# x times w_in2 by seven products of 2x2 blocks, and w_out2's parts from DRAM through a ring

## The chip, the cores and the metric
One Trainium2 chip, one of its cores. The metric is the device time of the kernel in microseconds. The engines are TensorE (PE; its weight loads are shown as PEld), VectorE (DVE), ScalarE (ACT), GpSimd (POOL) and SyncE (SP), which here issues all DMAs.

## The reference
```
attention, twice, for 8 batches x 8 heads (seq 576, head_dim 64, 32 packs):
    p_packed = softmax(p k^T / 8) v ;  a = softmax(q p_packed^T / 8) p_packed
x  = a, heads side by side                      (4608 tokens x 512)
h  = x @ w_in1 ;  g = h - tanh(h) ;             x1 = g @ w_out1   (512 -> 2048 -> 512)
h2 = x1 @ w_in2 ; g2 = s*relu(h2)^2 + b ;       y  = g2 @ w_out2  (512 -> 2048 -> 512)
```
All in float32. x1 and y are kept transposed, features on the partitions.

## The kernel before, in words
Every large product is made of three matmuls (`product`, lines 172 to 176). Each operand is split into a high part (rounded to the type in which TensorE takes a column per cycle) and a low part (the rest), and high*high, high*low and low*high are added up in PSUM. Each of the three brings its own 128 x 128 weights.

The work has two layers. The first (batches 0 to 7, two units of 288 tokens each, 16 units) holds the attention and the first pair of weights. The attention's second half is folded into the weights: m parts (`MB`) are the packed values times w_in1. A unit has 16 steps, one per chunk of 128 hidden features: `first1` makes the chunk (6 matmuls of 288 columns), ScalarE and VectorE make g and its two parts, and two steps later `second` multiplies them with w_out1 into four banks (12 matmuls). `side` puts the attention's small matmuls for the next batch behind fixed steps; step m counts 0 to 31 in a batch, and the loops of ScalarE and VectorE have the same steps written out. x1 goes to DRAM unit by unit (`store_x`).

The second layer has 9 blocks of 512 tokens, 16 steps each, 144 steps. A block's x1 is read back (`load_x`), and GpSimd splits it into parts (`split_x`), two blocks in turn. `first2` makes a chunk of h2 from the four row blocks of w_in2: 4 x 3 matmuls of 512 columns. ScalarE does relu (L656), VectorE the square (L923), ScalarE scale and bias (L659) and the high part (L663), VectorE the low part (L927). `second` multiplies with w_out2, 12 matmuls of 512 columns, two steps behind. All of w_in2 and w_out2 lies in SBUF as parts: w_in2 is loaded in batch 7 and split by ScalarE and VectorE, one piece of 512 columns per step (`high_w_in2`, `low_w_in2`); w_out2 is loaded into w_out1's place as that comes free, and GpSimd splits it (`split_w_out`).

The order on each engine is the program's order, and semaphores join them. TensorE's loop is

```
for c in range(STEPS + LAG):
    if c < STEPS1:
        first1(c)
        side(c)
    elif c < STEPS:
        first2(c)
    if c >= LAG:
        second(c - LAG)
```

Banks 0 to 3 hold the output of `second`, banks 4 and 5 the chunks of h in turn, banks 6 and 7 the attention's work.

## Time and profile before

| | us |
|---|---|
| median of 3 runs | 1506.68 (1506.4 to 1507.57) |
| the profiled execution | 1507.28, its span 1505.5 |
| TensorE busy | 1492.1 |
| VectorE busy | 642.9 |
| ScalarE busy | 611.7 |
| GpSimd busy | 158.0 |
| DMA, mean over the span | 50 GB/s, 75.43 MB |

The busy time of an engine adds up the time in which at least one of its instructions runs. Matmuls overlap, so the mean duration of one is longer than the time it adds. The first layer ends and the second begins at about 715 us of the span.

### The profile page before, as it was taken

Reading aid. Unit: us, or ns where it says so; the run is one execution under the profiler, and the core shown is the slowest. Engines: PE = TensorE matmul, PEld = TensorE weight load, DVE = VectorE, ACT = ScalarE, POOL = GpSimd, SP = SyncE. Lnnn points to the kernel's source line nnn. Section 1 sums busy time; section 2 is a strip of 40 time slices with the busy share of each in tenths; the row PEclk is TensorE's granted clock in tenths of the full one; section 3 lists DMA queues with packets and bytes.
Section 4 is the critical chain, followed back from the end, with each engine's and each line's share of the span. In section 5 each row is a group of like instructions: output and inputs, shape, how many; then the busy total and the mean of one; then the engine's idle time right before and its main releaser. Section 6 shows DMA issues by size and latency. Waiting matters only on the chain.

```text
span 1505.5 us, 23375 instructions
## 1 busy us (share of the span) xinstructions
PE 1492.1 (99%) x9852; PEld 1300.5 (86%) x9852; DVE 642.9 (43%) x1212; ACT 611.7 (41%) x1185; POOL 158.0 (10%) x95
## 2 busy tenths in 40 slices
PE   7999999999999999999999999999999999999999
PEld 5999989898998989899888888888888888888887
DVE  5755555555555555565333223232322323232222
ACT  3444344444444444454434333343334334333333
POOL 4600000000000000003912002020200202020000
PEclk9999999999999999999999999999999999999999
DMA  9402121120212110033201001010101001010000
GB/s 347 144 17 80 48 80 49 48 67 15 80 49 79 49 48 17 2 129 126 75 1 56 0 6 51 1 57 0 56 1 24 32 1 56 1 57 0 28 1 28
DMA packets 48888, 75.43 MB, mean 50 GB/s; under 512 B 1936, under 2 KB 26640, under 8 KB 48784
## 3 DMA queue, kind: packets, MB, share of 16 engines
q1 hardware_dynamic: 48784, 73.93, 14.9%
q8 instruction: 79, 1.29, 0.4%
q14 instruction: 25, 0.20, 0.0%
HBM read 55.05 MB, written 18.87 MB: 49 GB/s over the span
## 4 chain that ended last, share of the span: by engine, by line
PE 99%; DVE 1%; DMA 0%; issue 0%; ACT 0%; SPq 0%; DVEq 0%
PE banks L174 32%; PE banks L175 31%; PE banks L176 31%; PE banks L402 2%; PE banks L351 1%; PE banks L373 1%; PE banks L417 1%; PE banks L359 0%; DMA kT<-k_T 0%; PE banks L341 0%; PE banks L382 0%; PE banks L360 0%; DVE m_parts L733 0%; DVE g_low L888 0%; DVE probs L750 0%
## 5 line engine op out<-in xcount | busy, mean ns | idle before, releaser
L174 PE MATMUL banks<-g_high,w_out_parts 128*128 128x288 f32 (+1 forms) x1600 | 534.0, 334 | 1.3 <-DVE m_parts L733 1.3
L176 PE MATMUL banks<-g_high,w_out_parts 128*128 128x288 f32 (+1 forms) x1600 | 525.7, 329 | 0.0
L175 PE MATMUL banks<-g_low,w_out_parts 128*128 128x288 f32 (+1 forms) x1600 | 525.5, 328 | 0.0
L174 PEld LDWEIGHTS banks<-g_high,w_out_parts 128*128 128x128 f32 x1600 | 300.0, 187 | 62.3 <-issue 37.9
L175 PEld LDWEIGHTS banks<-g_low,w_out_parts 128*128 128x128 f32 x1600 | 300.4, 188 | 22.6
L176 PEld LDWEIGHTS banks<-g_high,w_out_parts 128*128 128x128 f32 x1600 | 300.3, 188 | 22.4
L923 DVE TENSOR_TENSOR g<-banks,g 128x512 f32<-128x512 f32 x144 | 99.6, 692 | 331.6 <-ACT g L656 331.6
L656 ACT ACTIVATE g<-banks 128x512 f32<-128x512 f32 x144 | 86.1, 598 | 366.3 <-PE banks L176 366.3
L176 PE MATMUL banks<-x_parts,w_in_parts 128*128 128x512 f32 x576 | 224.1, 389 | 0.0
L174 PE MATMUL banks<-x_parts,w_in_parts 128*128 128x512 f32 x576 | 224.1, 389 | 0.0
L175 PE MATMUL banks<-x_parts,w_in_parts 128*128 128x512 f32 x576 | 224.1, 389 | 0.0
L608 ACT ACTIVATE g<-banks 128x288 f32<-128x288 f32 x256 | 105.2, 411 | 287.0 <-PE banks L176 285.9
L847 DVE TENSOR_TENSOR g<-banks,g 128x288 f32<-128x288 f32 x256 | 117.1, 457 | 227.2 <-ACT g L608 226.0
L927 DVE TENSOR_TENSOR g_low<-g,g_high 128x512 fp32r<-128x512 f32 x144 | 118.8, 825 | 221.1 <-ACT g_high L663 221.1
L659 ACT ACTIVATE g<-g,small 128x512 f32<-128x512 f32 x144 | 117.5, 816 | 109.3 <-DVE g L923 109.3
L174 PE MATMUL banks<-probs2T_parts,m_parts 128*128 128x288 f32 x512 | 151.9, 297 | 5.4 <-DVE probs2T_parts L774 5.4
L292 POOL TENSOR_TENSOR x_parts<-x_raw,small 128x2048 fp32r<-128x2048 f32 (+1 forms) x12 | 33.0, 2747 | 1167.5 <-DMA x_raw<-x1T_scratch 1167.5
L629 ACT CAST g_high<-g 128x288 fp32r<-128x288 f32 x256 | 110.7, 433 | 101.5 <-DVE g L847 100.3
L888 DVE TENSOR_TENSOR g_low<-g,g_high 128x288 fp32r<-128x288 f32 x256 | 125.1, 489 | 62.4 <-ACT g_high L629 60.0
L175 PE MATMUL banks<-probs2T_parts,m_parts 128*128 128x288 f32 x512 | 151.7, 296 | 0.0
L176 PE MATMUL banks<-probs2T_parts,m_parts 128*128 128x288 f32 x512 | 151.0, 295 | 0.0
L176 PEld LDWEIGHTS banks<-x_parts,w_in_parts 128*128 128x128 f32 x576 | 108.1, 188 | 22.6
(85 smaller groups left out, 1188.9 us busy)
## 6 DMA issues: line engine op xcount, KB each, us to landing
kT<-k_T SPq DMA_DIRECT2D x16, 576.0 KB, 4.5
qT<-q_T SPq DMA_DIRECT2D x16, 576.0 KB, 6.0
x1T_scratch<-x_store SPq DMA_DIRECT2D x16, 576.0 KB, 3.4
x_raw<-x1T_scratch SPq DMA_DIRECT2D x9, 1024.0 KB, 6.5
v_rows<-v_rows SPq DMA_DIRECT2D x8, 1024.0 KB, 5.3
w_out_raw<-w_out SPq DMA_DIRECT2D x8, 1024.0 KB, 9.3
out_T<-y_store SPq DMA_DIRECT2D x8, 1024.0 KB, 8.7
w_in_rows<-w_in SPq DMA_DIRECT2D x4, 1024.0 KB, 13.2
```

Source lines behind the costliest of these rows:

```text
L174: nc.tensor.matmul(out, high, rhigh, start=first, stop=False)
L175: nc.tensor.matmul(out, high, rlow, start=False, stop=False)
L176: return nc.tensor.matmul(out, low, rhigh, start=False, stop=last)
L292: return nc.gpsimd.tensor_tensor(high, raw, ones, ALU.mult)
L608: nc.scalar.activation(TG1[:, c % 2, :], HB[:, c % 2, 0:U1], ACT.Tanh).then_inc(act_done, 1)
L629: nc.scalar.copy(GH1[:, c % RING, :], TG1[:, c % 2, :]).then_inc(high_done, 1)
L656: nc.scalar.activation(TG2[:, c % 2, :], HB[:, c % 2, :], ACT.Relu).then_inc(act_done, 1)
L659: nc.scalar.activation(TG2[:, c % 2, :], TG2[:, c % 2, :], ACT.Identity, bias=b_col, scale=s_col).then_inc(g_done, 1)
L847: nc.vector.tensor_tensor(TG1[:, c % 2, :], HB[:, c % 2, 0:U1], TG1[:, c % 2, :], ALU.subtract).then_inc(g_done, 1)
L888: nc.vector.tensor_tensor(GL1[:, c % RING, :], TG1[:, c % 2, :], read(GH1[:, c % RING, :]), ALU.subtract).then_inc(low_done, 1)
L923: nc.vector.tensor_tensor(TG2[:, c % 2, :], HB[:, c % 2, :], TG2[:, c % 2, :], ALU.mult).then_inc(r2_done, 1)
L927: nc.vector.tensor_tensor(GL2[:, c % RING, :], TG2[:, c % 2, :], read(GH2[:, c % RING, :]), ALU.subtract).then_inc(low_done, 1)
```

## The change
In the second layer, h2 = x1 w_in2 is computed by Strassen's scheme in Winograd's form on 2 x 2 blocks: w_in2 is cut into two halves of the contraction (256 rows each) by pairs of chunks (128 hidden features each), a block of x1 into the same two halves by two halves of its tokens (256 each). `seven` makes the seven products of a pair of chunks, each 2 x 3 matmuls of 256 columns, where two steps had 2 x 12 of 512. Products 1 to 4 go to the left halves of banks 4 to 7, 5 to 7 to the right halves of banks 4 to 6; each waits until its bank has been read. ScalarE copies product 1; VectorE adds the others up to the four blocks of h2 (c11, c12, c21, c22) and makes relu(h)*h in one operation per chunk.

The sums and differences of the blocks are made ahead and split: of w_in2 once, for each of 8 pairs of chunks (`mix_w_in2`, `high_w_in2`, `low_w_in2`), from step 5 of batch 7 to the fourth pair of the second layer; of x1 for each of the 9 blocks, by VectorE and ScalarE (`mix_x` at the fifth pair of the block before, `high_x` and `low_x` at its last), no longer by GpSimd. TensorE's order is seven(0), then seven(Q) ahead of the two `second2` of pair Q-1.

The parts of w_in2's combinations take w_out2's room. w_out2 is split by GpSimd through a staging tile, three chunks per batch in batches 1 to 6, and its parts are stored to DRAM. In the second layer a ring of four chunks (512 KB each) is refilled by SyncE, one chunk per step, each time a chunk has been used.

```diff
+PF = FC // 2
+U2H = U2 // 2
+NPR = 7
+PAIRS2 = NU2 * PF
...
+MIX_AT = {5: 0, 12: 1, 15: 2, 18: 3, 26: 4, 30: 5}
+SPLIT_AT = {7: (0, 0), 10: (0, 1), 13: (1, 0), 14: (1, 1), 16: (2, 0), 17: (2, 1), 19: (3, 0), 20: (3, 1),
+    27: (4, 0), 28: (4, 1), 31: (5, 0)}
+X_AT = {23: (0, 1), 25: (2, 3), 29: (4,), 30: (5,)}
+MIX2_AT = {0: 6, 2: 7}
+SPLIT2_AT = {0: ((5, 1),), 1: ((6, 0), (6, 1)), 2: ((7, 0),), 3: ((7, 1),)}
...
+    w2_dram = nc.dram_tensor("w_out2_parts_scratch", (FC, P, 2 * DM), F32).ap()
...
+    def split_w_out2(i):
+        wait(sp, w_out2_out, 16 * i)
+        sp.dma_start(STG_RAW[:, 1, :], w_out2[i, :, :]).then_inc(w_out2_raw_in, 16)
+        sp.wait_ge(w_out2_split, i + 1)
+        sp.dma_start(w2_dram[i, :, :].rearrange("p (a f) -> p a f", a=2), read(STG[:, :, :])
+                     ).then_inc(w_out2_out, 16)
+
+    def second_done(c):
+        unit, i = divmod(c, FC)
+        if i < FC - 1:
+            sp.wait_ge(g_used, (FC - 1) * unit + i + 1)
+        else:
+            sp.wait_ge(o_done, KX * (unit + 1))
+
+    def load_w_out2(cc):
+        sp.dma_start(read(WR[:, cc % RING, :, :]), w2_dram[cc % FC, :, :].rearrange("p (a f) -> p a f", a=2)
+                     ).then_inc(w_out2_in[cc % RING], 16)
+
...
+            for q in range(PF // 2):
+                load_w_in2(q)
+            sp.wait_ge(s2_done, NU1)
+            sp.wait_ge(x1_out, 32)
+            load_x(0)
...
+        if 1 <= b < B - 1:
+            for i in range(3 * b - 3, min(3 * b, FC)):
+                split_w_out2(i)
...
+    sp.wait_ge(w_out2_out, 16 * FC)
+    second_done(STEPS1 - FC + 1)
+    for cc in range(RING):
+        load_w_out2(cc)
+    for q, i in ((4, 5), (5, 8), (6, 12), (7, 15)):
+        second_done(STEPS1 - FC + i)
+        load_w_in2(q)
...
+    for Q in range(PAIRS2):
+        n, q = divmod(Q, PF)
+        if q == 0 and n + 1 < NU2:
+            sp.wait_ge(xo_ready, NPR * (n + 1))
+            load_x(n + 1)
+        for cc in (2 * Q + RING, 2 * Q + RING + 1):
+            if cc < 2 * PAIRS2:
+                second_done(STEPS1 + cc - RING)
+                load_w_out2(cc)
+        if q == 1 and n >= 1:
+            sp.wait_ge(o_copied_act, 2 * (NU1 + n))
+            sp.wait_ge(o_copied_dve, 2 * (NU1 + n))
+            sp.dma_start(outT[:, (n - 1) * U2:n * U2].rearrange("(d p) t -> p d t", p=P),
...
-        split_x(n)
+        pool.wait_ge(w_out2_raw_in, 16 * (i + 1))
+        split(STG[:, 0, :], STG[:, 1, :], STG_RAW[:, 1, :], 2 + FC + i + 1, w_out2_split)
...
+    def seven(Q):
+
+        n, q = divmod(Q, PF)
+        for j in range(NPR):
+            if n == 0:
+                pe.wait_ge(wc_ready, 2 * q + 1 + j // 4)
+            if q == 0:
+                pe.wait_ge(xo_ready, NPR * n + j + 1)
+            if j == 4:
+                pe.wait_ge(p1_copied, Q + 1)
+            elif j > 4:
+                pe.wait_ge(comb_done, NPR * Q + j - 4)
+            elif Q >= 1:
+                pe.wait_ge(comb_done, NPR * (Q - 1) + (4, 5, 7, 6)[j])
+            elif j == 0:
+                pe.wait_ge(g_done, STEPS1)
+            elif j == 2:
+                pe.wait_ge(dve_max2, 2 * (NU1 - 1))
+            out = banks[:, 4 + j % 4, (j // 4) * U2H:(j // 4 + 1) * U2H]
+            w = WC[q // 4][:, q % 4, j, :, :]
+            for kp in range(2):
+                cols = slice(kp * P, (kp + 1) * P)
+                last = product(out, w[:, 0, cols], w[:, 1, cols], XO[:, j, 0, kp, :], XO[:, j, 1, kp, :],
+                               kp == 0, kp == 1)
+            last.then_inc(prod_done, 1)
+
+    def second2(cc):
+
+        n, i = divmod(cc, FC)
+        pe.wait_ge(low_done, STEPS1 + cc + 1)
+        pe.wait_ge(w_out2_in[cc % RING], 16 * (cc // RING + 1))
+        for d in range(KX):
+            if i == 0:
+                pe.wait_ge((o_copied_act, o_copied_dve)[d % 2], 2 * (NU1 + n) - 1 + d // 2)
+            cols = slice(d * P, (d + 1) * P)
+            last = product(O[:, d, :], WR[:, cc % RING, 0, cols], WR[:, cc % RING, 1, cols],
+                           GH2[:, cc % RING, :], GL2[:, cc % RING, :], i == 0, i == FC - 1)
...
+    seven(0)
+    for Q in range(1, PAIRS2 + 1):
+        if Q < PAIRS2:
+            seven(Q)
+        second2(2 * Q - 2)
+        second2(2 * Q - 1)
...
+    def high_w_in2(q, part):
+        act.wait_ge(wc_mix, 4 * q + 3 + part)
+        rows = slice(0, 4) if part == 0 else slice(4, NPR)
+        nc.scalar.copy(WC[q // 4][:, q % 4, rows, 0, :], WC_RAW[q // 4][:, q % 4, rows, 1, :]
+                       ).then_inc(wc_high, 1)
+
+    def high_x(n, j):
+        if j in (0, 1, 4):
+            act.wait_ge(x_in, 16 * (n + 1))
+        else:
+            act.wait_ge(xt_done, 4 * n + {3: 1, 5: 2, 2: 3, 6: 4}[j])
+        if n == 0:
+            act.wait_ge(h_done, STEPS1 - FC + 4 * (j // 2) + 4)
+        else:
+            act.wait_ge(prod_done, NPR * (PF * n - 1) + j + 1)
+        nc.scalar.copy(XO[:, j, 0, :, :], x_raw(j)).then_inc(xo_high, 1)
...
+    high_x(0, 6)
     act.wait_ge(sb_in, 32)
...
+    for Q in range(PAIRS2):
...
+        act.wait_ge(prod_done, NPR * Q + 1)
+        if Q >= 1:
+            act.wait_ge(comb_done, NPR * (Q - 1) + 2)
+        nc.scalar.copy(C1[:, :], banks[:, 4, 0:U2H]).then_inc(p1_copied, 1)
+
+        if q == PF - 1 and n + 1 < NU2:
+            for j in range(NPR):
+                high_x(n + 1, j)
+
+        for k in range(2):
+            cc = 2 * Q + k
+            act.wait_ge(r2_done, cc + 1)
+            nc.scalar.activation(TG2[:, k, :], TG2[:, k, :], ACT.Identity, bias=b_col, scale=s_col
+                                 ).then_inc(g_done, 1)
+            act.wait_ge(g_done, STEPS1 + cc + 1)
+            nc.scalar.copy(GH2[:, cc % RING, :], TG2[:, k, :]).then_inc(high_done, 1)
+
+        for f, part in SPLIT2_AT.get(Q, ()):
+            high_w_in2(f, part)
...
+    def mix_w_in2(q):
+        w = WC_RAW[q // 4][:, q % 4, :, 1, :]
+        dve.wait_ge(wc_in[q], 32)
+        nc.vector.tensor_tensor(w[:, 3, :], w[:, 5, :], w[:, 6, :], ALU.add).then_inc(wc_mix, 1)
+        nc.vector.tensor_tensor(w[:, 5, :], w[:, 0, :], w[:, 5, :], ALU.subtract).then_inc(wc_mix, 1)
+        dve.wait_ge(wc_mix, 4 * q + 1)
+        nc.vector.tensor_tensor(w[:, 2, :], w[:, 3, :], w[:, 0, :], ALU.subtract).then_inc(wc_mix, 1)
+        dve.wait_ge(wc_mix, 4 * q + 3)
+        nc.vector.tensor_tensor(w[:, 4, :], w[:, 1, :], w[:, 2, :], ALU.subtract).then_inc(wc_mix, 1)
+
+    def low_w_in2(q, part):
+        dve.wait_ge(wc_high, 2 * q + part + 1)
+        dve.wait_ge(wc_mix, 4 * q + 4)
+        rows = slice(0, 4) if part == 0 else slice(4, NPR)
+        nc.vector.tensor_tensor(WC[q // 4][:, q % 4, rows, 1, :], WC_RAW[q // 4][:, q % 4, rows, 1, :],
+                                read(WC[q // 4][:, q % 4, rows, 0, :]), ALU.subtract).then_inc(wc_ready, 1)
...
+            wait(dve, xo_high, NPR * n)
+            nc.vector.tensor_tensor(TR[:, 0, :, :], b12, b11, ALU.subtract).then_inc(xt_done, 1)
+            nc.vector.tensor_tensor(TR[:, 1, :, :], b22, b12, ALU.subtract).then_inc(xt_done, 1)
+        else:
+            dve.wait_ge(xt_done, 4 * n + 1)
+            nc.vector.tensor_tensor(TR[:, 2, :, :], b22, TR[:, 0, :, :], ALU.subtract).then_inc(xt_done, 1)
+            dve.wait_ge(xt_done, 4 * n + 3)
+            nc.vector.tensor_tensor(TR[:, 3, :, :], TR[:, 2, :, :], b21, ALU.subtract).then_inc(xt_done, 1)
...
+    def low_x(n, j):
+        dve.wait_ge(xo_high, NPR * n + j + 1)
+        nc.vector.tensor_tensor(XO[:, j, 1, :, :], x_raw(j), read(XO[:, j, 0, :, :]), ALU.subtract
+                                ).then_inc(xo_ready, 1)
...
+        elif m in (21, 22):
+            mix_x(0, m - 21)
+        elif m in MIX_AT:
+            mix_w_in2(MIX_AT[m])
...
+        else:
+            if m in SPLIT_AT:
+                low_w_in2(*SPLIT_AT[m])
+            for j in X_AT.get(m, ()):
+                low_x(0, j)
...
+    low_x(0, 6)
+    for Q in range(PAIRS2):
...
+        dve.wait_ge(prod_done, own + 2)
+        dve.wait_ge(p1_copied, Q + 1)
+        plus(c11, C1[:, :], half(5, 0))
+        dve.wait_ge(prod_done, own + 3)
+        plus(u2, C1[:, :], half(6, 0))
+        dve.wait_ge(prod_done, own + 4)
+        dve.wait_ge(comb_done, own + 2)
+        plus(c12, u2, half(7, 0))
+        dve.wait_ge(prod_done, own + 5)
+        dve.wait_ge(comb_done, own + 3)
+        plus(c12, c12, half(4, 1))
+        dve.wait_ge(comb_done, own + 4)
+        if Q >= 1:
+            dve.wait_ge(high_done, STEPS1 + 2 * Q - 1)
+        nc.vector.scalar_tensor_tensor(TG2[:, 0, :], C[:, 0, :], 0.0, C[:, 0, :], ALU.max, ALU.mult
+                                       ).then_inc(r2_done, 1)
+        dve.wait_ge(prod_done, own + 6)
+        plus(u3, u2, half(5, 1))
+        dve.wait_ge(comb_done, own + 5)
+        plus(c22, u3, half(7, 0))
+        dve.wait_ge(prod_done, own + 7)
+        plus(c21, u3, half(6, 1), ALU.subtract)
+        dve.wait_ge(comb_done, own + 7)
+        if Q >= 1:
+            dve.wait_ge(high_done, STEPS1 + 2 * Q)
+        nc.vector.scalar_tensor_tensor(TG2[:, 1, :], C[:, 1, :], 0.0, C[:, 1, :], ALU.max, ALU.mult
+                                       ).then_inc(r2_done, 1)
+
+        if Q in MIX2_AT:
+            mix_w_in2(MIX2_AT[Q])
+        last_pair = q == PF - 1 and n + 1 < NU2
+        if last_pair:
+            low_x(n + 1, 0)
+            low_x(n + 1, 1)
+        low_g(2 * Q)
+        if last_pair:
+            low_x(n + 1, 2)
+            low_x(n + 1, 3)
+        low_g(2 * Q + 1)
+        if last_pair:
+            for j in (4, 5, 6):
+                low_x(n + 1, j)
+        for f, part in SPLIT2_AT.get(Q, ()):
+            low_w_in2(f, part)
+        if q == PF // 2 and n + 1 < NU2:
+            mix_x(n + 1, 0)
+            mix_x(n + 1, 1)
```

## Rows read from the trace of the kernel before

**Rows 1.** Page: busy time of engines; chain that ended last, by engine
```profile
PE 1492.1 (99%) x9852; PEld 1300.5 (86%) x9852; DVE 642.9 (43%) x1212; ACT 611.7 (41%) x1185; POOL 158.0 (10%) x95
...
PE 99%; DVE 1%; DMA 0%; issue 0%; ACT 0%; SPq 0%; DVEq 0%
```

**Rows 2.** Waits of TensorE: who waited for whom, us in total, times, longest
```profile
PE banks L174 <- DVE probs2T_parts L774: 5.4, 1, 5.4
PE banks L174 <- DVE m_parts L733: 1.3, 1, 1.3
```

**Rows 3.** Timeline (start us, duration us), ScalarE: first, last of 25, of 128
```profile
654.34 0.41 ACT L608 ACTIVATE g<-banks 128x288 f32<-128x288 f32 x1 [1.03 <-PE banks L176]
...
711.70 0.41 ACT L608 ACTIVATE g<-banks 128x288 f32<-128x288 f32 x1 [1.03 <-PE banks L176]
...
803.28 0.60 ACT L656 ACTIVATE g<-banks 128x512 f32<-128x512 f32 x1 [2.62 <-PE banks L176]
...
1494.16 0.60 ACT L656 ACTIVATE g<-banks 128x512 f32<-128x512 f32 x1 [2.62 <-PE banks L176]
```

**Rows 4.** Timeline of TensorE: after a break, and transposes
```profile
306.16 0.19 PEld L174 LDWEIGHTS banks<-g_high,w_out_parts 128*128 128x128 f32 x1 [0.47 <-issue]
306.16 0.40 PE L174 MATMUL banks<-g_high,w_out_parts 128*128 128x288 f32 x1
306.27 0.19 PEld L175 LDWEIGHTS banks<-g_low,w_out_parts 128*128 128x128 f32 x1
...
141.05 0.60 PE L359 MATMUL banks<-identity,probs 128*128 128x128 f32 x4
141.48 0.27 PE L360 MATMUL banks<-identity,probs 128*64 128x128 f32 x1
```

**Rows 5.** VectorE by line, shape: busy us, mean ns, idle before, releaser
```profile
L927 DVE TENSOR_TENSOR g_low<-g,g_high 128x512 fp32r<-128x512 f32 x144 | 118.8, 825 | 221.1 <-ACT g_high L663 221.1
...
L923 DVE TENSOR_TENSOR g<-banks,g 128x512 f32<-128x512 f32 x144 | 99.6, 692 | 331.6 <-ACT g L656 331.6
...
L824 DVE TENSOR_TENSOR w_in_parts<-w_in_raw,w_in_parts 128x512 fp32r<-128x512 f32 x16 | 10.8, 677 | 0.0
...
L741 DVE TENSOR_TENSOR m_parts<-banks,m_parts 128x256 fp32r<-128x256 f32 x1 | 0.4, 418 | 0.0
```

**Rows 6.** ScalarE by line and shape
```profile
L659 ACT ACTIVATE g<-g,small 128x512 f32<-128x512 f32 x144 | 117.5, 816 | 109.3 <-DVE g L923 109.3
...
L663 ACT CAST g_high<-g 128x512 fp32r<-128x512 f32 x144 | 89.3, 620 | 4.5
...
L551 ACT COPY probs<-banks 128x288 f32<-128x288 f32 x14 | 5.5, 392 | 0.0
```

**Rows 7.** Timeline of VectorE in batch 7: two operations in a row
```profile
676.65 0.68 DVE L824 TENSOR_TENSOR w_in_parts<-w_in_raw,w_in_parts 128x512 fp32r<-128x512 f32 x1
677.25 0.45 DVE L888 TENSOR_TENSOR g_low<-g,g_high 128x288 fp32r<-128x288 f32 x1
```

**Rows 8.** Timeline near 1000 us: GpSimd and VectorE
```profile
997.86 4.94 POOL L306 TENSOR_TENSOR x_parts<-x_raw,x_parts 128x2048 fp32r<-128x2048 f32 x1
...
1001.99 1.37 DVE L927 TENSOR_TENSOR g_low<-g,g_high 128x512 fp32r<-128x512 f32 x1 [1.54 <-ACT g_high L663]
```

**Rows 9.** Window: PE, PEld, DVE, ACT, POOL busy us (count); clock, DMA, GB/s
```profile
25.00:60.00 35.00, 33.56 (x293) 28.79 (x286) 28.59 (x44) 16.30 (x39) 33.58 (x27) 0.97 0.73 255
```

**Rows 10.** DMA issues: size, us to landing; w_in2's four loads, their landing
```profile
x1T_scratch<-x_store SPq DMA_DIRECT2D x16, 576.0 KB, 3.4
x_raw<-x1T_scratch SPq DMA_DIRECT2D x9, 1024.0 KB, 6.5
...
out_T<-y_store SPq DMA_DIRECT2D x4, 256.0 KB, 2.0
...
644.27 3.21 SPq L207 DMA_DIRECT2D w_in_raw<-w_in  x4
...
DMA to landing us min/median/max: 6.5/9.4/12.2
```

More of the change, by code:

```diff
@@ L141, in build @@
     w_in1_in = [sem(f"w_in1_in{i}") for i in range(NB)]
[L142 removed]
+    wc_in = [sem(f"w_in2_in{q}") for q in range(PF)]
     w_out1_in = [sem(f"w_out1_in{i}") for i in range(4)]
[L144 to L145 removed]
+    w_out2_in = [sem(f"w_out2_in{i}") for i in range(RING)]
+    w_out2_raw_in, w_out2_split, w_out2_out = sem("w_out2_raw_in"), sem("w_out2_split"), sem("w_out2_out")
+    x_in = sem("x_in")
     zeroed, ident_ready = sem("zeroed"), sem("ident_ready")
@@ L176, in product, with x_raw @@
         return nc.tensor.matmul(out, low, rhigh, start=False, stop=last)
+    def x_raw(j):
+        if j in (0, 1, 4):
+            kh, th = ((0, 0), (1, 0), None, None, (1, 1))[j]
+            return XR[:, 2 * kh:2 * kh + 2, th * U2H:(th + 1) * U2H]
+        return TR[:, {3: 0, 5: 1, 2: 2, 6: 3}[j], :, :]
     block = nc.Block()
@@ L225, in _ @@
             load_w_in1(0)
-            load_w_out(0, w_out1, w_out1_in)
+            load_w_out1(0)
             load_w_in1(1)
@@ L247, in _ @@
                     sp.wait_ge(m_done, NB * B)
-                    for k in range(KX):
-                        load_w_in2(k)
+                    for q in range(PF // 2):
[3 more added lines that the diff above has]
+                    load_x(0)
                 if b + 2 < B:
@@ L438, in first1, with second1 @@
                 last.then_inc(h_done, 1)
-            def first2(c):
-                n, i = divmod(c - STEPS1, FC)
-                if i == 0:
-                    pe.wait_ge(xb_ready, KX + n)
-                if c == STEPS1:
-                    pe.wait_ge(w_in2_ready, KX * NB)
-                pe.wait_ge(g_done, c - 1)
-                for k in range(KX):
-                    cols = slice(k * FF + i * P, k * FF + (i + 1) * P)
-                    last = product(HB[:, c % 2, :], WIN[:, 0, cols], WIN[:, 1, cols],
-                                   XB[:, n % 2, 0, k, :], XB[:, n % 2, 1, k, :], k == 0, k == KX - 1)
-                last.then_inc(h_done, 1)
-            def second(c):
+            def second1(c):
                 unit, i = divmod(c, FC)
-                width, ring_high, ring_low, ready = (U1, GH1, GL1, w_out1_ready) if c < STEPS1 else \
-                    (U2, GH2, GL2, w_out2_ready)
                 pe.wait_ge(low_done, c + 1)
-                pe.wait_ge(ready, i + 1)
+                pe.wait_ge(w_out1_ready, i + 1)
                 if c == 0:
@@ L466, in second @@
                     cols = slice(d * P, (d + 1) * P)
-                    last = product(O[:, d, 0:width], WOUT[:, 0, i, cols], WOUT[:, 1, i, cols],
-                                   ring_high[:, c % RING, :], ring_low[:, c % RING, :], i == 0, i == FC - 1)
+                    last = product(O[:, d, 0:U1], WOUT[:, i, 0, cols], WOUT[:, i, 1, cols],
+                                   GH1[:, c % RING, :], GL1[:, c % RING, :], i == 0, i == FC - 1)
+                    if i == FC - 1:
+                        last.then_inc(o_done, 1)
+                    elif d == KX - 1:
+                        last.then_inc(g_used, 1)
@@ L528, in _ @@
             m_block(0, 0)
-            for c in range(STEPS + LAG):
+            for c in range(STEPS1 + LAG):
                 if c < STEPS1:
@@ new lines, in half, with plus, low_g @@
+            def half(b, h):
+                return banks[:, b, h * U2H:(h + 1) * U2H]
+            def plus(out, a, p, op=ALU.add):
+                nc.vector.tensor_tensor(out, a, p, op).then_inc(comb_done, 1)
+            def low_g(cc):
+                dve.wait_ge(high_done, STEPS1 + cc + 1)
+                nc.vector.tensor_tensor(GL2[:, cc % RING, :], TG2[:, cc % 2, :], read(GH2[:, cc % RING, :]),
+                                        ALU.subtract).then_inc(low_done, 1)
+            low_x(0, 6)
@@ new lines, in _ @@
+            for Q in range(PAIRS2):
+                n, q = divmod(Q, PF)
+                own = NPR * Q
+                if Q == 0:
+                    for d in (1, 3):
+                        copy_o(NU1 - 1, d, OS1, U1, x1_out, 16 * (NU1 - 1))
+                if q == 1 and n >= 1:
+                    for d in (1, 3):
+                        copy_o(NU1 + n - 1, d, OS2, U2, y_out, 16 * (n - 1))
+                c11, c12, c21, c22 = (C[:, k, h * U2H:(h + 1) * U2H] for k in range(2) for h in range(2))
+                u2, u3 = U[:, 0, :], U[:, 1, :]
+                dve.wait_ge(prod_done, own + 2)
[44 more added lines that the diff above has]
+                    mix_x(n + 1, 1)
```

182 lines of the change are left out of this document (67 added, 115 removed).

## The prediction
> **What bounds the kernel now.** I read the page first: TensorE is busy 99% of the span and 99% of the chain that ended last runs through it [rows 1]. The waits of TensorE add up to 10.9 us, the two longest are 5.4 and 1.3 us, and by the lines that end them all belong to the first layer [rows 2]. So a change counts by what it does to TensorE's own time, unless it makes TensorE wait. What one matmul costs there is not its busy mean (matmuls overlap) but its slot, the distance to the next one. It is read from the rhythm of ScalarE's first operation on each step, which starts when a step's hidden columns are done [rows 3]. In the first layer 24 steps take 57.36 us, 2.390 us each; a step has 6 + 12 matmuls of 288 columns, so a slot is 0.1328 us. In the second layer 127 steps take 690.88 us, 5.440 us each for 12 + 12 matmuls of 512 columns: 0.2267 us. Both are 0.013 us above the time of the columns at the granted 2.4 GHz (0.120 and 0.2133 us).
>
> **TensorE's work after the change.** The unit is a pair of chunks (two steps). Before, a pair is 48 matmuls of 512 columns, 10.88 us; the half that multiplies with w_out2 stays (24, 5.44 us). The other half becomes 7 products x 2 halves of the contraction x 3 parts = 42 matmuls of 256 columns. No row of the second layer shows this width. The line through the two slots of rows 3 has (0.2267 - 0.1328)/224 = 0.00042 us per column and gives 0.1328 - 32 x 0.00042 = 0.1194 us. 42 x 0.1194 = 5.01 us against 5.44: 0.43 us less per pair, and over 72 pairs 30.7 us less.
> That is small, since 18 more slots pay the fixed 0.013 us, and it hangs on the slot. Upper bound: every matmul here brings its own weights, and if 0.1328 were the least that a weight load allows, 42 slots would take 5.58 us, 9.9 us more over the kernel than before. Lower bound: after a break in the first layer two weight loads start 0.11 us apart, with no matmul ahead of them, and four transposes with 128 columns and 128 weights each follow each other every 0.108 us [rows 4]; a slot as short as 0.110 us gives 4.62 us, 59 us less over the kernel. I take the line: 0.1194 lies above what rows 4 need for the weights, and the excess over the columns was the same at both widths.
> The Trainium skill ("TensorE: Matmul & The Clock Gate", section "Back-to-back issue gap") has columns / 2.4 + 2.5 ns for the slot, which would be 0.109 us here and a saving of 61 us instead of 30.7. The trace disagrees at both widths that it has: 0.1328 against the rule's 0.1225 and 0.2267 against 0.2158 [rows 3]. Its figure for a load of 128 weights (same page, "LDWEIGHTS (loading the stationary operand)") is 107 ns, and there the trace agrees with 0.11 us [rows 4].
>
> **The other engines, per pair.** VectorE now forms h from the products: 7 operations on 256 columns at about 0.42 us, two squares with relu on 512 columns (an operation that no row shows; between 0.68 and 0.83 us by the two-input operations of that width, I take 0.69, the row that reads PSUM, as it is also what an undisturbed row of the SBUF form takes), and two low parts at 0.69 [rows 5]. One that waits for nothing starts 0.08 us before the last one's end [rows 7]. That is 5.0 to 5.7 us in a pair of 10.45. ScalarE copies the first product (0.37 us by the copy of 288 columns), and twice scales (0.82) and casts (0.62): 3.3 us [rows 6]. The relu on ScalarE goes. GpSimd's splits of x go with the whole second layer's use of it: a low part beside one took 1.37 us instead of 0.69 [rows 8]. None of this was on TensorE's path, so it counts nothing.
>
> **Waits inside a pair.** Count from the end of a pair's seven products, T. A product is seen about 0.19 us after its last slot (its last matmul outlasts its slot by about 0.16). Product 5 writes the bank of product 1 and waits for ScalarE's copy; product 6 waits for c11, product 7 for u2. Product 2 is seen 1.6 us after the seven begin, c11 is done at 2.05, product 6 is due at 3.6: 1.5 us to spare, if VectorE is free. It is: after T the order is u3, c22, c21 (to T+1.05), the second square (T+1.8), ScalarE's scale and cast of it (T+3.3), low parts (T+2.4 to 4.3). The next seven begin at T+5.44, since the 24 matmuls with w_out2 lie between. At the fifth pair of a block (512 tokens) four mixes of x follow, 2.7 us, to T+7: still ahead of T+8.6, when c11 must start.
> At the last pair of a block seven high parts (ScalarE) and seven low parts (VectorE) of the next x are added. ScalarE follows the products: 0.62 against 0.72 us each, the last one at T+0.8. VectorE's order is u3, c22, c21, square, two low x, low g, two, low g, three; at 0.6 to 0.69 us each it ends at T+7.2, then c11 at T+7.6, due T+9.0. The low parts are due from T+5.4 on, one every 0.72 us, and come from T+2.4 on. I count nothing; without the overlap of rows 7 and with the 0.83 us mean of the low parts [rows 5] it would be T+9.4 for the low parts, and c11 0.8 us late, at 8 edges.
> The start of the layer has no such cover: seven(1) follows seven(0) at once. ScalarE finishes the casts of pair 0 at T+3.25 and one weight split (768 columns, about 0.8 us), only then copies product 1: done T+4.4 where product 5 is due at T+2.9, 1.6 us lost. VectorE has the second square, four mixes of w_in2, two low parts and a weight split (about 0.9): c11 at T+5.8, due 5.2, 0.6 us lost. 2.2 us once.
>
> **Work moved into the first layer.** Batch 7 had 16 high and 16 low parts of w_in2 of 512 columns; now VectorE has 5 mixes of four 256-column operations before step 27 (about 1.5 us each), splits of 1024 and 768 columns (1.2 and 0.9), mixes and low parts of x. Between steps 12 and 23, the densest, this is 15 us beside 9 us of its own work, in 28.7 us of TensorE's. It fits; I allow 0.5 us for a step that is late. The splits of w_out2 go to batches 1 to 6, sixteen times two GpSimd operations. In the stretch where GpSimd did the same for w_out1 (27 operations in 35 us) VectorE's 44 operations took 0.65 us each, longer than alone, yet TensorE was busy 33.56 of 35 us, and the 1.3 us wait in it is for an m part [rows 9, 2]. SyncE stops at each split, 2.0 us of load for 256 KB, two GpSimd operations at 33.58/27 = 1.24 us, 3.4 of store for 512 to 576 KB, 8 us, 24 for three [rows 9, 10]. Only the store of x of that batch is queued behind; it goes out near step 27 instead of 17, and its buffer is written again at step 33, 14 us later. Nothing.
>
> **The ring.** Each chunk's 512 KB goes out when the chunk four before it is used, and it is due 2.72 + 5.01 + 5.44 + 5.01 = 18.2 us later. Beside it the queue holds at worst one more chunk and a transfer of 1 MB. Four loads of 1 MB issued within 3.2 us landed 6.5 to 12.2 us after their issue, one x load took 6.5 [rows 10]. So 2 MB is there in about 9 us, and the ring hides. Its 75 MB make about 100 GB/s over the layer; the start had 255 GB/s beside matmuls [rows 9].
>
> **Sum.** The profiled execution took 1507.28 us, 1.78 more than its span and 0.6 more than the median. 1507.28 - 30.7 + 2.2 + 0.5 = 1479.3; by the median 1478.7. I say 1479.
>
> **Rivals.**
> (a) VectorE is late at the block edges or by one operation more in each pair, because the unseen square or the waits between dependent operations are dearer. 1 to 2 us at 8 edges make 1487 to 1495. For it: the mean of 0.83 us. Against: it contains GpSimd's share, which goes. 19%.
> (b) The slot has a floor of 0.1328 us from its own weights. 9.9 + 2.7 us over before: 1519. For it: no row has a shorter slot of this kind. Against: the 0.11 us of rows 4, and the same excess at 512 columns, where weights can't bind. 6%.
> (c) The chain product 2, c11, product 6 is late in each pair, from behind VectorE's earlier work. It decides from 1.5 us of delay on and eats the gain from 0.43 us of stall per pair, 1.9 us of delay; at 1 us of stall it is 1479 + 72 = 1551. Against: VectorE is about half idle. Slower than before 5%, in part (1496 to 1505) 4%, at no change 2%.
> (d) A slot near 0.110 us, which the weights allow: 1507 - 59 + 2.7 = 1451. Against: the constant excess. 4%.
> The Trainium skill's slot rule (same page and section as above) would put it there too, at 1449; the trace does not follow it.
> (e) The ring is late: from 18 us of landing on each microsecond counts per chunk. It belongs with (c) by size, and rows 10 leave it half of that; it is in (c)'s share.
>
> **The numbers.** Forecast 60% (1475 to 1484), rivals as given. Faster by over 0.2% (3 us, about what a measurement of this kernel can tell): 60 + 19 + 4 + 4 = 87%; within 2%; slower 6 + 5 = 11%. The range takes forecast and (a): 1473 to 1496.
>
> **What would show it.** Right: a pair lasts 10.45 us in steady state, by the starts of ScalarE's copy of product 1; the 256-column matmuls start 0.119 us apart; TensorE's waits name VectorE's c11 or ScalarE's copy at pair 1 alone, some 2 us; GpSimd is still after batch 6; batches 1 to 6 keep their length. Wrong: slots of 0.13 us between the seven; waits on the combining lines every pair or every eighth pair; low x waits; a wait on the ring's loads.

## The result: 1482.18 us, 1.7% less, and the profile after

The changed kernel takes 1482.18 us (median of 4 runs, 1481.46 to 1482.29) where the kernel before took 1507.12 beside it (4 runs, 1506.40 to 1508.70). The ratio is 0.9832, with a 95% interval of 0.9815 to 0.9849. The forecast was 1479. The profiled execution took 1481.46 us with a span of 1479.7, 25.8 us less than before in both.

Busy time of the engines on the page after, against [rows 1]:

```profile
PE 1463.2 (99%) x11148; PEld 1337.7 (90%) x11148; DVE 902.5 (61%) x1847; ACT 594.8 (40%) x1176; POOL 79.9 (5%) x71
```

VectorE has 260 us more to do and the kernel is faster: TensorE is as full as before, and its own time fell by 28.9 us.

The rhythm is read as in [rows 3], now from ScalarE's copy of product 1, of which each pair of chunks has one. These are the copies of pair 3 and pair 71 (counted from 0) in the timeline after:

```profile
747.28 0.37 ACT L752 COPY p_copy<-banks 128x256 f32<-128x256 f32 x1 [2.17 <-PE banks L204]
...
1461.28 0.37 ACT L752 COPY p_copy<-banks 128x256 f32<-128x256 f32 x1 [3.12 <-PE banks L204]
```

714.00 us for 68 pairs are 10.50 us each, against 10.88 for two steps before. Every one of the 68 is 10.50: no block edge, no fifth pair stands out.

The slot of the new width, from TensorE's timeline after (first, tenth after it):

```profile
999.80 0.28 PE L202 MATMUL banks<-x_operands,w_in_first 128*128 128x256 f32 x1
...
1001.00 0.28 PE L203 MATMUL banks<-x_operands,w_in_first 128*128 128x256 f32 x1
```

Ten slots are 1.20 us: 0.120 us each. The waits of TensorE after, with those that answer to [rows 2] first:

```profile
PE banks L202 <- DVE probs2T_parts L871: 5.4, 1, 5.4
PE banks L202 <- DVE m_parts L830: 1.7, 1, 1.7
PE banks L202 <- ACT p_copy L752: 1.4, 1, 1.4
...
PE banks L202 <- DVE h L1060: 0.4, 1, 0.4
```

Two waits are new, each once. The timeline at the start of the second layer shows them in order (SyncE's, VectorE's low parts and TensorE's other rows left out):

```profile
719.01 0.37 ACT L752 COPY p_copy<-banks 128x256 f32<-128x256 f32 x1 [0.72 <-PE banks L204]
...
726.28 0.83 ACT L664 CAST w_in_last<-w_in_raw_last 128x768 fp32r<-128x768 f32 x1
...
727.02 0.36 ACT L752 COPY p_copy<-banks 128x256 f32<-128x256 f32 x1
...
727.47 0.95 DVE L934 TENSOR_TENSOR w_in_last<-w_in_raw_last,w_in_last 128x768 fp32r<-128x768 f32 x1
...
727.53 0.36 PE L202 MATMUL banks<-x_operands,w_in_first 128*128 128x256 f32 x1 [1.36 <-ACT p_copy L752]
...
728.33 0.41 DVE L1060 TENSOR_TENSOR h<-p_copy,banks 128x256 f32<-128x256 f32 x1
...
728.89 0.35 PE L202 MATMUL banks<-x_operands,w_in_first 128*128 128x256 f32 x1 [0.42 <-DVE h L1060]
...
736.78 0.37 ACT L752 COPY p_copy<-banks 128x256 f32<-128x256 f32 x1 [0.89 <-PE banks L204]
```

ScalarE's copy of pair 1 (727.02) starts right behind the weight split (726.28), and TensorE's product 5 behind the copy. The price of both waits is read from the copies of pairs 0 and 2: they are 736.78 - 719.01 = 17.77 us apart. Without a wait the distance would be 42 slots for the seven products of pair 1, which follow those of pair 0 at once, and then one ordinary pair: 5.04 + 10.50 = 15.54. The waits cost 2.2 us.

VectorE's operations after, by line and shape, against [rows 5]:

```profile
L1064 DVE TENSOR_TENSOR g_low<-g,g_high 128x512 fp32r<-128x512 f32 x144 | 98.9, 688 | 58.1 <-ACT g_high L764 58.1
...
L1105 DVE SCALAR_TENSOR_TENSOR g<-h 128x512 f32<-128x512 f32 x72 | 50.0, 694 | 2.4
...
L1060 DVE TENSOR_TENSOR h<-p_copy,banks 128x256 f32<-128x256 f32 x72 | 30.4, 422 | 149.3 <-PE banks L204 149.3
```

The low part fell from a mean of 825 to 688 ns, with GpSimd still. In the trace before, the 22 of its 144 low parts that had an operation of GpSimd beside them took 1561 ns on average, the other 122 took 692: the mean of [rows 5] was high through those 22 alone. The unseen square takes 694.

### The profile page after: what moved, and what is told of

It is laid out like the page before. It is cut to its first block, busy times and chain, and to the rows that moved or that the text cites. A ratio compares the mean times of both kernels' runs of the same rounds, so it can differ in the third digit from the quotient of the medians.

```text
span 1479.7 us, 27233 instructions
## 1 busy us (share of the span) xinstructions
PE 1463.2 (99%) x11148; PEld 1337.7 (90%) x11148; DVE 902.5 (61%) x1847; ACT 594.8 (40%) x1176; POOL 79.9 (5%) x71
## 4 chain that ended last, share of the span: by engine, by line
PE 97%; DVE 2%; DMA 0%; ACT 0%; issue 0%; SPq 0%; DVEq 0%
PE banks L202 31%; PE banks L203 31%; PE banks L204 30%; PE banks L442 2%; PE banks L413 1%; PE banks L391 1%; PE banks L457 1%; PE banks L399 1%; DMA kT<-k_T 0%; DVE g_low L1020 0%; DVE m_parts L830 0%; PE banks L422 0%; PE banks L400 0%; DVE probs L900 0%; DVE h L1060 0%
## 5 line engine op out<-in xcount | busy, mean ns | idle before, releaser
L202 PE MATMUL banks<-g_high,w_out_parts 128*128 128x288 f32 x1024 | 309.9, 303 | 1.7 <-DVE m_parts L830 1.7
L204 PE MATMUL banks<-g_high,w_out_parts 128*128 128x288 f32 x1024 | 301.6, 295 | 0.0
L203 PE MATMUL banks<-g_low,w_out_parts 128*128 128x288 f32 x1024 | 301.4, 294 | 0.0
L202 PEld LDWEIGHTS banks<-g_high,w_out_parts 128*128 128x128 f32 x1024 | 192.0, 187 | 40.2 <-issue 33.6
L202 PE MATMUL banks<-g_high,w_out_ring 128*128 128x512 f32 x576 | 225.0, 391 | 0.0
L203 PE MATMUL banks<-g_low,w_out_ring 128*128 128x512 f32 x576 | 224.9, 391 | 0.0
L204 PE MATMUL banks<-g_high,w_out_ring 128*128 128x512 f32 x576 | 224.1, 389 | 0.0
L204 PEld LDWEIGHTS banks<-g_high,w_out_parts 128*128 128x128 f32 x1024 | 192.3, 188 | 0.0
L203 PEld LDWEIGHTS banks<-g_low,w_out_parts 128*128 128x128 f32 x1024 | 192.2, 188 | 0.0
L1020 DVE TENSOR_TENSOR g_low<-g,g_high 128x288 fp32r<-128x288 f32 x256 | 129.9, 507 | 66.1 <-ACT g_high L718 63.9
L202 PE MATMUL banks<-x_operands,w_in_first 128*128 128x256 f32 x504 | 142.6, 283 | 1.8 <-ACT p_copy L752 1.4
L204 PE MATMUL banks<-x_operands,w_in_last 128*128 128x256 f32 x504 | 142.6, 283 | 0.0
L204 PE MATMUL banks<-x_operands,w_in_first 128*128 128x256 f32 x504 | 142.6, 283 | 0.0
L203 PE MATMUL banks<-x_operands,w_in_last 128*128 128x256 f32 x504 | 142.6, 283 | 0.0
L203 PE MATMUL banks<-x_operands,w_in_first 128*128 128x256 f32 x504 | 142.6, 283 | 0.0
```

The lines of the kernel that those rows point to most:

```text
L202: nc.tensor.matmul(out, high, rhigh, start=first, stop=False)
L203: nc.tensor.matmul(out, high, rlow, start=False, stop=False)
L204: return nc.tensor.matmul(out, low, rhigh, start=False, stop=last)
L1020: nc.vector.tensor_tensor(GL1[:, c % RING, :], TG1[:, c % 2, :], read(GH1[:, c % RING, :]), ALU.subtract).then_inc(low_done, 1)
```

## The experiments

**The ring alone.** The kernel before, with w_out2 split in batches 1 to 6 and streamed; x times w_in2 untouched.

```diff
+                w = WOUT[:, i, :, :] if c < STEPS1 else WR[:, cc % RING, :, :]
...
-                    last = product(O[:, d, 0:width], WOUT[:, 0, i, cols], WOUT[:, 1, i, cols],
+                    last = product(O[:, d, 0:width], w[:, 0, cols], w[:, 1, cols],
```

> The kernel before with the second part of the change alone: w_out2 is split through the staging tile in batches 1 to 6, its parts go to DRAM, and the second layer reads them through the ring of four chunks; x times w_in2 stays as it was, 12 matmuls of 512 columns per step. Theory (TensorE's slots alone make the time, all else is hidden): no change, within 1 us of before, a step of 5.44 us and a TensorE that waits nowhere in the second layer. Rival (the ring's 75 MB disturb the matmuls with w_out2, whose slot was 0.2275 us after the change against 0.2267 before): a step of 5.46 us, 3 us longer than before. Rival (part of the gain came from taking work off GpSimd and out of w_out2's late split): some us faster than before.

1507.02 us (10 runs) against 1507.21, ratio 0.9999, 0.9989 to 1.0009. Two steps 127 apart in its timeline:

```profile
802.74 0.60 ACT L686 ACTIVATE g<-banks 128x512 f32<-128x512 f32 x1 [2.62 <-PE banks L181]
...
1493.62 0.60 ACT L686 ACTIVATE g<-banks 128x512 f32<-128x512 f32 x1 [2.62 <-PE banks L181]
```

5.440 us a step, as before to the last digit. The ring and its 120 GB/s cost nothing and bring nothing by themselves that these runs could tell (0.1%), and neither does having w_out2 split before the second layer begins. By the code, the ring is what makes room in SBUF for the combinations of w_in2.

**The ring without its traffic.** The changed kernel with small refills: most of each chunk of w_out2 is left out.

```diff
-                        load_w_out2(cc)
+                        load_small(cc)      # 32 of 1024 columns
```

> The changed kernel, with the ring's loads after the first four cut from 512 KB to 16 KB each (it leaves out the refill, so the products with w_out2 use old chunks). If the ring's traffic lengthens the slots of the matmuls (0.2275 us against 0.2267 before, 0.12 against the line's 0.1194): a pair of 10.45 instead of 10.50 us, 3.6 us less, 1478.6. If the traffic costs nothing: 1482 as with it, a pair of 10.50 us.

1482.21 us (4 runs), and a pair of 10.50 us (69 in a row), with the core's DMA at 32 instead of 129 GB/s between 800 and 1100 us. The traffic does not explain that a pair is 10.50 and not the 10.45 of the forecast.

**Half width, no scheme.** The kernel before with twice as many, half as wide matmuls of x times w_in2.

```diff
-                for k in range(KX):
-                    cols = slice(k * FF + i * P, k * FF + (i + 1) * P)
-                    last = product(HB[:, c % 2, :], WIN[:, 0, cols], WIN[:, 1, cols],
-                                   XB[:, n % 2, 0, k, :], XB[:, n % 2, 1, k, :], k == 0, k == KX - 1)
+                for t in (slice(0, 256), slice(256, 512)):
+                    for k in range(KX):
+                        cols = slice(k * FF + i * P, k * FF + (i + 1) * P)
+                        last = product(HB[:, c % 2, t], WIN[:, 0, cols], WIN[:, 1, cols],
+                                       XB[:, n % 2, 0, k, t], XB[:, n % 2, 1, k, t], k == 0, k == KX - 1)
```

> The kernel before, with each matmul of 512 columns of x times w_in2 made as two of 256 (the same columns and sums, no block scheme, same weights twice). Theory (a slot is its columns plus a fixed 0.0133 us): 24 more slots per two steps, 24 x 0.0133 = 0.32 us per pair of steps, a step of 5.60 us, 1507 + 23 = 1530 us. Rival (the second matmul with the same weights is cheaper than one with new ones): between 1507 and 1530.

1531.95 us (one run). Steps of 5.62 us (88 of them from 1024.24 to 1518.80), 11.24 per pair: 0.36 more than before for 24 more slots with the same columns. The price of a matmul beyond its columns is real: 0.36/24 = 0.015 us, near the 0.0133 expected. 48 x 0.120 + 24 x 0.2267 explain 11.20, and 0.04 was over. The rival, a cheaper second matmul with the same weights, is not really tested: in this order the same weights come back only 12 matmuls later.

**The same, grouped.** Two steps' products of x with w_in2 first, then two steps' products of g with w_out2. A change of kind below is a change from matmuls of 256 columns to those of 512, or back.

```diff
-                elif c < STEPS:
-                    first2(c)
+                elif c < STEPS and c % 2 == 0:
+                    first2(c)
+                    first2(c + 1)
```

> The kernel before with each matmul of x times w_in2 as two of 256 columns, and two steps grouped: 48 matmuls of 256, then 24 of 512, as the changed kernel alternates (one change from one kind to the other and back per pair of steps, where the ungrouped version had two). If each change of kind costs 0.01 us: a pair of 48 x 0.120 + 24 x 0.2267 + 0.02 = 11.22 us against 11.24 ungrouped. If instead the slot at 256 columns is 0.1208 us and a change of kind costs nothing: 11.24 us. Both differ by 1.4 us in the sum, too little for the time alone; the rhythm of ScalarE's first operation in the trace tells it.

1530.54 us (one run). Two pairs 44 apart:

```profile
1018.11 0.60 ACT L658 ACTIVATE g<-banks 128x512 f32<-128x512 f32 x1 [5.51 <-PE banks L176]
...
1511.79 0.60 ACT L658 ACTIVATE g<-banks 128x512 f32<-128x512 f32 x1 [5.52 <-PE banks L176]
```

493.68/44 = 11.22 us. Half of the changes of kind gave back half of the 0.04 us, and 1.4 us between the two single runs. So a change of kind costs 0.01 us on average, and the changed kernel, with two per pair, has 42 x 0.120 + 24 x 0.2267 + 0.02 = 10.50: its rhythm, to the digit.

TensorE's own timeline of the changed kernel shows where the 0.02 us lie. These are the first two matmuls of a pair's seven products, the first and the sixth of the matmuls with w_out2 behind them, and the first of the next seven:

```profile
998.37 0.28 PE L202 MATMUL banks<-x_operands,w_in_first 128*128 128x256 f32 x1
998.48 0.28 PE L203 MATMUL banks<-x_operands,w_in_first 128*128 128x256 f32 x1
...
1003.40 0.40 PE L202 MATMUL banks<-g_high,w_out_ring 128*128 128x512 f32 x1
...
1004.56 0.39 PE L204 MATMUL banks<-g_high,w_out_ring 128*128 128x512 f32 x1
...
1008.87 0.28 PE L202 MATMUL banks<-x_operands,w_in_last 128*128 128x256 f32 x1
```

The first five slots of 512 columns take 1.16 us instead of 1.133, all later ones 0.2267; the first slot of 256 is 0.11 instead of 0.120. Averaged over 62 pairs of this trace, the way up to 512 columns costs 0.0275 us, spread over five matmuls, and the way down gives 0.0075 back. The slots of both half-width versions have the same pattern, so it comes neither from the block scheme nor from the ring.

**The floor of a slot.** The changed kernel with 35 of 42 matmuls at 128 columns.

```diff
-                        last = product(out, w[:, 0, cols], w[:, 1, cols], XO[:, j, 0, kp, :], XO[:, j, 1, kp, :],
-                                       kp == 0, kp == 1)
+                        for a, b in ((0, 0), (0, 1), (1, 0)):
+                            n_cols = U2H if (kp, a, b) == (0, 0, 0) else P
+                            last = nc.tensor.matmul(out[:, 0:n_cols], w[:, a, cols], XO[:, j, b, kp, 0:n_cols], ...)
```

> The changed kernel, with 35 of the 42 matmuls of the seven products cut to 128 of 256 columns (it leaves out part of the products' sums). It measures what was unseen in the prediction: how short a slot can be when each matmul brings its own 128 x 128 weights. Columns plus 0.0133 us: slot 0.0667 us, seven products in 7 x 0.120 + 35 x 0.0667 = 3.17 us, a pair of 8.63 us, 1482 - 72 x 1.87 = 1347 us. A floor of 0.108 us from the weights: 4.62 us, a pair of 10.08, 1452 us. A floor at 0.120 us (the width of 256 is already bound by the weights): no change, 1482.

1462.82 us (one run). Its copies of product 1, 67 pairs apart:

```profile
760.31 0.37 ACT L754 COPY p_copy<-banks 128x256 f32<-128x256 f32 x1 [2.25 <-PE banks L524]
...
1442.82 0.37 ACT L754 COPY p_copy<-banks 128x256 f32<-128x256 f32 x1 [2.98 <-PE banks L524]
```

10.187 us a pair. The 24 matmuls with w_out2 take more of it than before, since the change of kind costs more from 128 columns; these are the first and the last of them in one pair:

```profile
906.78 0.45 PE L202 MATMUL banks<-g_high,w_out_ring 128*128 128x512 f32 x1
...
912.06 0.39 PE L204 MATMUL banks<-g_high,w_out_ring 128*128 128x512 f32 x1
```

With the last slot of 0.227 they take 5.51 us. That leaves 4.68 for the 42, and without 7 x 0.120 the 35 narrow slots took 3.84 us, 0.110 us each. (Between two others of 128 columns a narrow slot is 0.112 us on average in this trace.) Their columns alone would be 0.053. On average a slot with its own 128 weights doesn't get shorter than 0.11 us here, the distance that the weight loads of [rows 4] had. At 256 columns (0.120) the kernel stands about 0.01 us above it.

The whole is 11 us longer than the 1452 expected. 8 us of it are the pair, 10.187 instead of 10.08. Another part is pair 1, which the expectation did not count: with shorter products the same waits are a little longer there, and the granted clock fell behind them to 1.2 GHz (0.50). Two rows of the waits, and the stretch behind them (length, busy us (instructions) of PE, PEld, DVE, ACT, POOL, then granted clock, DMA share and GB/s):

```profile
PE banks L524 <- ACT p_copy L754: 1.6, 1, 1.6
...
PE banks L524 <- DVE h L1062: 0.5, 1, 0.5
...
731.60:735.00 3.40, 3.40 (x13) 2.82 (x12) 3.30 (x7) 1.99 (x3) 0.00 (x0) 0.50 0.00 0
```

The copies of pairs 0 and 2 are 19.05 us apart, where 4.68 + 10.19 = 14.87 would be the distance without a wait: 4.2 us lost instead of 2.2.

**The first pair's waits.** First w_in2's late mix and splits moved back by a pair or two; then besides at pair 1 the copy and the first two sums moved ahead of pair 0's second chunk.

```diff
-MIX2_AT = {0: 6, 2: 7}
-SPLIT2_AT = {0: ((5, 1),), 1: ((6, 0), (6, 1)), 2: ((7, 0),), 3: ((7, 1),)}
+MIX2_AT = {1: 6, 3: 7}
+SPLIT2_AT = {1: ((5, 1),), 2: ((6, 0), (6, 1)), 4: ((7, 0),), 5: ((7, 1),)}
```

> The changed kernel, with the mix and the splits of w_in2 that lie behind pairs 0 to 3 of the second layer moved to pairs 1 to 5. Theory (at pair 1 product 5 waits for ScalarE's copy, which stands behind the split of pair 0, then product 6 for VectorE's c11 behind four mixes, 2.2 us in all): without them the copy is done at 3.6 us after seven(1) begins where product 5 is due at 2.9, and c11 at 4.8 where product 6 is due at 4.3: 1.3 us lost instead of 2.2, so 0.9 us faster than the changed kernel, which is at the edge of what can be measured; the pairs' rhythm in the trace shows it. Rival (the 2.2 us come from the switch of the first layer to the second, not from this queue): no change of the distance from pair 0's to pair 2's copy, 17.8 us.

1480.27 us (4 runs). The copies of pairs 0 and 2 stand at 718.71 and 735.16, 16.45 us apart: 1.3 us less, where 0.9 was expected; product 5 still waits 0.6 us for the copy. The rival (the switch of layers) would have left 17.8.

```diff
+                    if cc == 0:
+                        copy_p1(1)
...
+                if Q == 1:
+                    low_g(1)
```

`copy_p1(1)` stands behind ScalarE's cast of chunk 0, `low_g(1)` behind VectorE's u2 of pair 1; each is left out at its usual place.

> The same, and besides, at pair 1 alone, ScalarE copies product 1 before the second chunk of pair 0 is scaled and cast, and VectorE makes c11 and u2 before the second low part of pair 0. Theory: the copy is done 1.8 us after seven(1) begins, c11 at 2.8, both before they are due; no wait of TensorE in the second layer, seven(1) as long as all others, 2.2 us faster than the changed kernel (about 1480). Rival (a wait comes up at the next place, second2(1) for its late low part): the 2.2 us stay in part. It would be the fastest version.

1478.89 us (5 runs), ratio 0.9819 to before, 0.9806 to 0.9833: the lowest median of all versions. Its interval overlaps that of the changed kernel, so the times alone don't separate them; the trace does:

```profile
718.67 0.37 ACT L742 COPY p_copy<-banks 128x256 f32<-128x256 f32 x1 [0.72 <-PE banks L204]
...
724.11 0.36 ACT L742 COPY p_copy<-banks 128x256 f32<-128x256 f32 x1
...
734.21 0.37 ACT L742 COPY p_copy<-banks 128x256 f32<-128x256 f32 x1 [1.77 <-PE banks L204]
```

15.54 us between the first and the last, the distance without a wait; its span is 1477.1 us, 2.6 less than 1479.7 (0.3 of it ahead of the first copy, outside this edit), and TensorE waits nowhere in the second layer.

**How much cover c11 has.** Three, then six more operations of VectorE at the end of each pair.

```diff
+                wait(dve, spare_done, 3 * Q)
                 plus(c11, C1[:, :], half(5, 0))
...
+                for e in range(3):
+                    wait(dve, spare_done, 3 * Q + e)
+                    nc.vector.tensor_tensor(C[:, 0, :], C[:, 1, :], C[:, 1, :], ALU.mult).then_inc(spare_done, 1)
```

> The changed kernel with 3 more operations of VectorE at the end of every pair, each 512 columns wide and waiting for the last (0.73 us each, 2.2 us), to measure how much cover c11 has. By the order worked out: ordinary pairs are free at 6.5 us after the seven products where c11 must start by 8.6, no loss; at the fifth pair of a block 7.0 + 2.2 + 0.4 against 9.0, 0.6 late, and at the last pair 7.2 + 2.2 + 0.4, 0.8 late; 8 blocks x 1.4 = 11 us, 1493. If VectorE's time were worth anything by itself: 72 x 2.2 = 158 us. If the cover is larger than worked out: 1482.

1495.13 us (one run). Three copies in its timeline, the last one at a block edge:

```profile
1134.61 0.37 ACT L753 COPY p_copy<-banks 128x256 f32<-128x256 f32 x1 [3.12 <-PE banks L205]
...
1145.11 0.37 ACT L753 COPY p_copy<-banks 128x256 f32<-128x256 f32 x1 [2.76 <-PE banks L205]
...
1156.54 0.37 ACT L753 COPY p_copy<-banks 128x256 f32<-128x256 f32 x1 [0.80 <-PE banks L205]
```

Ordinary pairs stay at 10.50, edges are 11.43 (0.93 late, 0.8 expected), the pair after the mixes of x 10.71 (0.2, where 0.6 was expected). 8 x 1.15 = 9 us; another 3.6 us are at pair 1, 13.33 us instead of 9.76, which I had not counted. There TensorE waits 2.7 us for c11 instead of 0.4, and the rest is the clock, as shown below. Adding three operations to each pair raised VectorE's busy time by 140.6 us (902.5 to 1043.1) and cost 13: VectorE's time is worth nothing until c11 is late.

The version with six has `6 * Q` and `range(6)` in the same places.

> The same with 6 more operations (4.4 us a pair, VectorE then at about 10 of 10.5 us). Ordinary pairs: free at 8.7, c11 0.1 late or not late; the fifth and the last pair of a block some 2.8 and 3.0 us late, and what they leave behind carries over: 8 x 5.8 = 46 us and up to 10 more, 1528 to 1540. If VectorE's sum alone decided (below 10.5 us, so hidden): 1482.

1584.84 us (one run), far above 1540. The order was right: pairs of mostly 16.7 us at the edges, 15.1 after the mixes, 10.5 to 11 else. So were the waits, nearly: c11 holds TensorE up by 2.8 us after the mixes and by 3.4 at the edges, where 2.8 and 3.0 were expected, and all its waits for c11 together are the first row here. Two of them stand under it:

```profile
PE banks L203 <- DVE h L1061: 63.0, 36, 4.9
...
1011.60 0.36 PE L203 MATMUL banks<-x_operands,w_in_first 128*128 128x256 f32 x1 [3.36 <-DVE h L1061]
...
1393.41 0.55 PE L203 MATMUL banks<-x_operands,w_in_first 128*128 128x256 f32 x1 [3.36 <-DVE h L1061]
```

63.0 us against 46 to 56 expected, but the span is 103 us longer than the changed kernel's. Most of what is over is the clock. Two stretches of its trace, in the columns as above:

```profile
1354.00:1356.00 2.00, 0.00 (x0) 0.00 (x0) 1.93 (x3) 0.00 (x0) 0.00 (x0) 1.00 0.00 0
...
1359.00:1362.00 3.00, 3.00 (x9) 2.34 (x9) 2.14 (x5) 2.56 (x4) 0.00 (x0) 0.59 0.00 0
```

and TensorE's timeline there:

```profile
1353.66 0.28 PE L205 MATMUL banks<-x_operands,w_in_last 128*128 128x256 f32 x1
1356.70 0.39 PE L203 MATMUL banks<-x_operands,w_in_last 128*128 128x256 f32 x1 [2.76 <-DVE h L1061]
...
1358.79 0.63 PE L204 MATMUL banks<-g_low,w_out_ring 128*128 128x512 f32 x1
1359.21 0.63 PE L205 MATMUL banks<-g_high,w_out_ring 128*128 128x512 f32 x1
```

From one matmul to the next over the wait for c11 it is 3.04 us, and soon after it the matmuls of 512 columns follow each 0.42 us instead of 0.227: the clock was at 1.2 instead of 2.4 GHz for a few us. So a wait of that size can cost a second time. In the second layer of this run the granted clock was at 1.2 GHz for 75 us in 16 stretches; at half speed they cost half of that, about 37 us by this estimate, and with the 62.6 us of longer waits for c11 that is 100 of the 103. The mean clock of the run is 0.974, against 0.998. The fall did not follow every such wait: behind the 3.36 us at 1011.60 the next 12 us ran at the full clock, behind the 3.36 us at 1393.41 they did not. The three-operation version shows the fall once, at its longest wait (pair 1), which is about 1.3 of the 3.6 us.

## Why the prediction was right, point by point

**TensorE's slots.** The mechanism was right: fewer columns, more slots, nothing else on the path. The size was 3.3 us off. Of the 30.7 us that it gave, 72 x 0.38 = 27.4 came. The term was the slot, read from a line through two widths: 0.1200 and not 0.1194 (72 x 42 x 0.0006 = 1.8 us). The line itself was sound, but one of its two points was not: 0.1328 for 288 columns is a mean over steps, and TensorE's timeline before has slots of two lengths in it. From the first to the second of these rows are 21 slots, from the third to the fourth is one:

```profile
656.52 0.29 PE L174 MATMUL banks<-g_high,w_out_parts 128*128 128x288 f32 x1
...
659.32 0.29 PE L174 MATMUL banks<-g_high,w_out_parts 128*128 128x288 f32 x1
...
659.85 0.29 PE L175 MATMUL banks<-g_low,w_out_parts 128*128 128x288 f32 x1
659.97 0.29 PE L176 MATMUL banks<-g_high,w_out_parts 128*128 128x288 f32 x1
```

2.80/21 = 0.1333 us, and of 36 slots (two steps) three are like the last one, 0.127 by the unrounded starts. Through 0.1333 the same line gives 0.1200 at 256 columns, as measured. Why those three are shorter stays open. The rest is the change from one kind of matmul to the other, 0.01 us each on average, two per pair, 1.4 us, which no term held. The half-width versions show both apart from the scheme and from the ring.

**The bounds of the slot.** The upper one (0.1328, rival b) is out by the slot in the trace. The lower one, 0.110, was right as a floor: 0.110 to 0.112 measured at 128 columns. It is no price for 256 columns, because there the columns and the fixed 0.0133 us last longer; rival (d) fell. So did the Trainium skill's gap of columns / 2.4 + 2.5 ns ("TensorE: Matmul & The Clock Gate", section "Back-to-back issue gap"): 0.109 against 0.120 measured. The Trainium skill gives that formula in this section for an isolated matmul and says that at few columns it is too short for a stream that loads weights for each, so the prediction took it for more than it claims. By the Trainium skill's columns / 1.2 for a load of weights (same page, "LDWEIGHTS (loading the stationary operand)") 128 columns are an estimated 107 ns, and the measured floor agrees to within 0.005 us.

**Waits in a pair and at the edges.** There was no wait from pair 2 on, as worked out; rivals (a) and (c) did not come. At an edge VectorE's timeline after reads:

```profile
799.28 1.29 DVE L954 TENSOR_TENSOR x_operands<-t_rows,x_operands 128x512 fp32r<-128x512 f32 x2
800.50 0.42 DVE L1060 TENSOR_TENSOR h<-p_copy,banks 128x256 f32<-128x256 f32 x1
```

ScalarE sees product 1 of the next pair at 799.78, which puts T, the end of the seven products before it, at 793.4; the low parts end at T+7.2 and c11 at T+7.5, where the order on paper had 7.2 and 7.6. c11 starts 0.72 us behind the copy of product 1, as in an ordinary pair: it waited for product 2 and not for the low parts. What carried the forecast were the right operation times: the row of the low part undisturbed by GpSimd, not its mean.

**The start of the layer.** 2.2 us forecast (1.6 for the copy, 0.6 for c11), 2.2 measured, and taken away by moving exactly the operations named.

**Work moved into the first layer, ring, GpSimd.** Counted at nothing but 0.5 us, and that was not needed: TensorE was busy 18.00 of 18 us at the end of batch 7, and the whole first layer ran 0.57 us ahead of the kernel before, the same from step 11 to its end. That difference arises in the first steps, outside the change, and it lies within what comes and goes by chance: in the changed kernel and the five versions that do the same work up to there (small refills, later splits, first pair, three and six operations) the first copy of product 1 starts anywhere from 718.50 to 719.91 us. A chunk of the ring landed 3.2 us after its issue (median of 144), with 18 us to go.

**The sum.** -27.4 + 2.2 - 0.6 = -25.8 us, the difference of the spans. Forecast: -30.7 + 2.2 + 0.5 = -28.0. The slots were 3.3 us off. The first layer was 1.1 us off the other way, 0.6 of it by chance, and so the sum was off by 2.2 only.

## What to carry to other kernels

Read what a matmul costs from a rhythm that repeats, not from its duration, and within a row of matmuls of one kind: a mean over whole steps hid three shorter slots in 36 and put the forecast 1.8 us off. Take the slot apart into columns and a fixed part: here 0.0133 us per matmul, so that a scheme which takes 1536 of 24576 columns (6%) out of a pair but makes nearly two thirds of its matmuls half as wide keeps 3.5%. Before trusting a narrower tile, find the floor that the weights set (0.11 us for 128 x 128 here). Where another engine gets much more to do, lay its order out against the due times at the places that differ from the rule (first pair, block edge); its total tells nothing until one operation is late, and then a long wait can cost twice, through the clock.
